# Scores and softmax of the windowed attention issued one half step earlier in the fused kernel

## The chip, the cores and the metric

The kernel runs on one core of a Trainium2 chip. Engines: TensorE (PE; its weight loads are listed as PEld), VectorE (DVE), ScalarE (ACT), GpSimd (POOL), SyncE (SP, which issues most DMAs). The metric is the device time of one execution in microseconds, as the median of several runs.

## The reference

A sliding-window attention, a dense layer with x - tanh(x), and a mixture of 8 experts in which each row goes to one expert:

```python
# q, k, v: (4, 8, 576, 64)
scores = (q @ k.T) / sqrt(64);  mask: 0 <= i - j < 64
attn = softmax(scores, axis=-1)          # row max subtracted, sum + 1e-9
x = (attn @ v) as (2304, 512) rows
h = x @ w_in                             # (512, 2048)
x = (h - tanh(h)) @ w_out                # (2048, 512)
# experts: unit rows of x against unit embeddings, / tau, argmax, softmax gate
out[mask] = gate[mask] * (relu(x[mask] @ w1[e]) @ w2[e])   # w1 512x1024, w2 1024x512
```

## The kernel before

Every product in fp32 accuracy is made of three matmuls of a high and a low part (`products`). The work has two phases: attention with the dense layer (to about 530 us), then the experts.

**Attention** comes in 48 groups. A group is one window of three 64-row blocks of one pair of heads. Its stages are, with their engines: `transpose_qk` (PE, line 1181) turns q and k; `evacuate` (DVE, 861 to 867) copies the turned q into the block-diagonal `qbd`, copies the last key block of the window before to the front of `kT` where the window does not start a sequence (the carry, 865), and copies the three new key blocks (867); `score` (PE, 1192) multiplies them; `mask_max` (DVE, 872) adds the mask and takes the maximum; `exp` (ACT, 654); `pad_sum` and `invert` (DVE, 879, 883); `normalise` (POOL, 521); `transpose_p` (PE, 1203); `copy_pT` (ACT, 661); `attend` (PE, 1219); `copy_x` (ACT, 670); `split_x` (POOL, 530 and 532) makes the high and low part of x.

**The dense layer** is done in 6 blocks of 384 rows. A block has 16 steps, c = 0 to 15, each of 128 hidden columns. In a step TensorE does `first_product(c)` (12 matmuls, x by w_in) and `second_product(c-2)` (9 matmuls, g by w_out). Between them `tanh` (ACT, 703), `less_tanh` (DVE, 954), `high_g` (ACT, 710) and `low_g` (DVE, 958) make g = h - tanh(h) and its two parts. `high_g` waits until the second product that used the same buffer is done.

**The first 8 groups** run before the dense layer. The other 40 are woven into its steps by hand. Each step has two slots: `pieces(s)` after the first product and `pieces(s + 1)` after the second. On VectorE and ScalarE the same slots are after `less_tanh` or `tanh`, and after `low_g` or `high_g`. Group g begins in a slot given by `first_slot`: every third slot for groups 8 to 15, every fourth for 16 to 47, and for the latter it is always the second slot of an even step. In that slot stand its transposes and its evacuation. The later stages stand a fixed number of slots (a lag) behind: score and mask_max at `LAG_SCORE` = 2, exp at 3, pad, reciprocal and normalise at 4, transpose_p at 6, attend and copy_x at 7, split_x at 8. Each engine executes its list in order; semaphores between engines make it wait where something is not there. Within one slot TensorE's order is attend, transpose_p, score, transpose_qk, of different groups. A `score` waits for `qk_evacuated`, which is raised by the key copy (867).

From the second block on VectorE also does the dot products of the router (`dot`, line 975) at the end of steps 3 to 11, four in an odd and one in an even step. In step 14 TensorE ranks rows (`rank`), in step 15 GpSimd scatters slots.

Of the kernel before, what the change touches and what calls it, by code (L numbers as in the profile page):

```python
# [14 lines left out]
BANK = 512  # L15
WINDOW = 64
MASKED = -1.0e30
LAG_SCORE, LAG_TURN, LAG_ATTEND = 2, 6, 7


def wait(eng, semaphore, value):
# [13 lines left out]
def build(nc, q, k, v, w_in, w_out, emb, tau, w1, w2, out):  # L35
# [30 lines left out]
    with ExitStack() as ctx:  # L66
# [254 lines left out]
        def begun(s, lag):  # L321

            return begins.get(s - lag)
# [171 lines left out]
        def _(pool):  # L495
# [23 lines left out]
            def normalise(g):  # L519
                pool.wait_ge(inverted, g + 1)  # L520
                pool.tensor_tensor(sm[g % 4][:], sm[g % 4][:], rr[:, g % 4, :].unsqueeze(2).broadcast_to((P, GB, P)),  # L521
                                   ALU.mult).then_inc(normed, 1)

            def split_x(g):

                n, kk, a = g // FIRST, pair_of(g), g % 2
                high, raw, low = (x[:, kk, n % 2, a, :] for x in (xh, xraw, xl))
                done = g if g < FIRST // 2 else g - FIRST // 2
                pool.wait_ge(x_copied, g + 1)
                pool.tensor_copy(high, raw).then_inc(x_high, 1)  # L530
                pool.wait_ge(x_high, done + 1)
                pool.tensor_tensor(low, raw, high, ALU.subtract).then_inc(x_split, 1)
# [48 lines left out]
                    split_x(j - 6)  # L581

            def pieces(s):
                if (g := begun(s, LAG_SCORE + 2)) is not None:
                    normalise(g)
                if (g := begun(s, LAG_ATTEND + 1)) is not None:
                    split_x(g)

            for n in range(NBLK):
                for c, s in steps(n):  # L590
                    if n == 0 and c + 2 < FC:
                        split_w_in(c + 2)
                    pieces(s)
                    pieces(s + 1)
                    if n == 0 and c in (3, 5):
                        constants(1 if c == 3 else 2)
                    if n == 0 and c == 6:
                        pool.wait_ge(en_squared, 1)
                        pool.tensor_tensor(enroot[:], en1[:, 0:1], power[0:E, 0:1], ALU.pow).then_inc(en_rooted, 1)
                    if n > 0 and c == 8:  # L600
                        pool.wait_ge(squared, ST * n)
                        pool.tensor_tensor(norm[:], ss[:], power[:], ALU.pow).then_inc(rooted, 1)
                    if n > 0 and c == 15:
                        scatter_slots(n - 1)
# [45 lines left out]
        def _(act):  # L650
            def exp(g):
                act.wait_ge(maxed, g + 1)
                for u in range(GB):
                    last = act.activation(sm[g % 4][:, u, :], sm[g % 4][:, u, :], ACT.Exp, bias=nmx[:, g % 4, u:u + 1],
                                          scale=-1.0, accum_out=rs[:, g % 4, u:u + 1])
                last.then_inc(exped, 1)

            def copy_pT(g):
                act.wait_ge(p_transposed, g + 1)
                wait(act, attended, g - 1)  # L660
                act.copy(pT[g % 2][:], psP(g)).then_inc(pT_copied, 1)

            def copy_x(g):
                n, kk, a = g // FIRST, pair_of(g), g % 2
                act.wait_ge(attended, g + 1)

                wait(act, h_ready, FC * (n - 1))
                for h in range(2):
                    rows = slice(h * D, (h + 1) * D)
                    last = act.copy(xraw[rows, kk, n % 2, a, :].rearrange("p (g c) -> p g c", g=GB),  # L670
                                    psO(g)[rows, :, h * WINDOW:(h + 1) * WINDOW])
                last.then_inc(x_copied, 1)
# [15 lines left out]
                    copy_x(j - 5)  # L688

            def pieces(s):  # L690
                if (g := begun(s, LAG_SCORE + 1)) is not None:
                    exp(g)
                if (g := begun(s, LAG_TURN)) is not None:
                    copy_pT(g)
                if (g := begun(s, LAG_ATTEND)) is not None:
                    copy_x(g)
# [35 lines left out]
            for n in range(NBLK):  # L732
                for c, s in steps(n):
                    if n > 0 and c == 2:
                        copy_acc(n - 1)
                    tanh(n, c)
                    pieces(s)
                    high_g(n, c)
                    pieces(s + 1)
                    if n == 0:  # L740
                        high_w_out(c)
                    if n > 0 and c in (3, 5, 7):
                        square(n - 1, (c - 3) // 2)
                    if n > 0 and c == 14:
                        exp_gate(n - 1)
# [97 lines left out]
        def _(dve):  # L843
# [10 lines left out]
            def evacuate(g):  # L854
                i, hp = g % 2, pair_of(g)
                dve.wait_ge(qk_transposed, g + 1)

                wait(dve, scored, g - 1)
                for h in range(2):
                    rows = slice(h * D, (h + 1) * D)  # L860
                    dve.tensor_scalar(qbd[i][rows, :, h, :], psT(g)[rows, :, 0:WINDOW], float(D) ** -0.5, None, ALU.mult)
                wait(dve, scored, g if g % 2 else g - FIRST + 2)
                if window_of(g) % GP:
                    carries[0] += 1
                    dve.tensor_copy(kT[hp][:, 0, :], kT[hp][:, GB, :]).then_inc(carried, 1)
                    dve.wait_ge(carried, carries[0])
                dve.tensor_copy(kT[hp][:, 1:1 + GB, :], psT(g)[:, :, WINDOW:P]).then_inc(qk_evacuated, 1)

            def mask_max(g, units):

                for u in units:
                    last = dve.tensor_tensor_reduce(sm[g % 4][:, u, :], psS(g)[:, u, :], (mask0 if window_of(g) % GP == 0 and u == 0 else mask)[:],
                                                    -1.0, -2.0 * MASKED, ALU.add, ALU.min, nmx[:, g % 4, u:u + 1])
                if units[-1] == GB - 1:
                    last.then_inc(maxed, 1)

            def pad_sum(g):
                dve.wait_ge(exped, g + 1)
                dve.tensor_scalar(rse[:, g % 4, :], rs[:, g % 4, :], 1e-9, None, ALU.add).then_inc(sum_padded, 1)

            def invert(g):
                dve.wait_ge(sum_padded, g + 1)
                dve.reciprocal(rr[:, g % 4, :], rse[:, g % 4, :]).then_inc(inverted, 1)  # L883
# [41 lines left out]
            def pieces(s):  # L925
                if (g := begun(s, 0)) is not None:
                    evacuate(g)
                if (g := begun(s, LAG_SCORE + 2)) is not None:
                    pad_sum(g)
                    invert(g)  # L930
                if (g := begun(s, LAG_SCORE)) is not None:
                    dve.wait_ge(scored, g + 1)
                    dve.wait_ge(p_transposed, g - 3)
                    mask_max(g, [0, 1, 2])
# [84 lines left out]
            for n in range(NBLK):  # L1019
                for c, s in steps(n):  # L1020
                    if n > 0 and c == 2:
                        copy_acc(n - 1)
                    less_tanh(n, c)
                    pieces(s)
                    low_g(n, c)
                    pieces(s + 1)
                    if n > 0 and c == 13:
                        choose(n - 1, dots[:])
                    if n > 0 and c == 15:
                        place(n - 1)  # L1030
                    if n > 0 and 3 <= c <= 11:

                        done = (c - 3) // 2 * 5 + (0 if c % 2 else 4)
                        for r in range(done, done + (4 if c % 2 else 1)):
                            dot(n - 1, r // ST, r % ST)
                    if n == 0:
                        low_w_out(c)
                    if n == 0 and c == 6:
                        scale_emb()
                    if n == 0 and c == 8:  # L1040
                        dve.wait_ge(en_transposed, 1)
                        dve.tensor_copy(enT[:].rearrange("p k e -> p (k e)"), banks[:, 7, 0:KC * E]).then_inc(en_ready, 1)
# [7 lines left out]
            def low_first_w1(pieces):  # L1050
                low_pieces(w1raw, w1h, w1l, ds(0, 1), w1_high, w1_split, 0, pieces)
# [421 lines left out]
```

## Time and profile before

| | us |
|---|---|
| median of 3 runs | 849.17 (849.06 to 849.85) |
| the profiled execution: its time, its span | 849.17, 847.0 |
| TensorE busy | 804.4 (95%) |
| VectorE busy | 468.0 (55%) |
| ScalarE busy | 368.0 (43%) |
| GpSimd busy | 200.5 (24%) |

The page cuts the span in 40 slices. TensorE is at nine tenths or more in nearly all of them, save the first, the change from the dense layer to the experts near 550 us, and the last. Durations of rows that follow each other on TensorE overlap, since matmuls are pipelined: what a matmul takes from the engine is the distance between the starts of two rows. The shares of VectorE and the others say little, for it counts only whether TensorE waits for them.

### The profile page before, as it was taken

The numbers are of one execution on the slowest core, as the hardware profiler recorded it, in microseconds if no ns is written. First come the engines' busy times: TensorE is split into PE (matmuls) and PEld (weight loads), VectorE is DVE, ScalarE is ACT, GpSimd is POOL, SyncE is SP. The second block draws the span as 40 slices with busy tenths as digits, with TensorE's granted clock in tenths as the row PEclk, the third lists the DMA queues.
The fourth block names the chain that finished last, engine by engine and source line by source line (L and its number), as shares of the span: only waits on it lengthen the run. The fifth ranks groups of instructions, "written<-read, shape, count | busy, mean of one in ns | idle before, by whom it ended". The sixth has DMA issues, their size and how long they took to land. (4 is left out here: it accounts for less than half of the span.)

```text
span 847.0 us, 16644 instructions
## 1 busy us (share of the span) xinstructions
PE 804.4 (95%) x4680; PEld 694.5 (82%) x4681; DVE 468.0 (55%) x1399; ACT 368.0 (43%) x910; POOL 200.5 (24%) x276
## 2 busy tenths in 40 slices
PE   7899999999999999999999998399999999999992
PEld 6888888888888888888889997278888888888871
DVE  7666645765577567756763665645443251654322
ACT  4554544433443344344442324246444442664333
POOL 4457621223122312131211001301111111111111
PEclk9999999999999999999999999599999999999995
DMA  9972123322332233223206211056271523466110
GB/s 176 238 232 67 40 51 100 76 61 49 99 79 56 50 100 85 52 50 100 69 14 224 75 38 38 27 202 221 73 236 47 185 93 121 152 236 225 49 47 17
DMA packets 106310, 87.87 MB, mean 104 GB/s; under 512 B 79012, under 2 KB 80169, under 8 KB 106242
## 3 DMA queue, kind: packets, MB, share of 16 engines
q1 hardware_dynamic: 98386, 74.92, 30.6%
q0 software_dynamic: 4624, 11.32, 4.4%
q10 hardware_dynamic: 3232, 0.79, 0.5%
q8 instruction: 35, 0.57, 0.3%
q14 instruction: 33, 0.27, 0.1%
HBM read 152.87 MB, written 11.46 MB: 194 GB/s over the span
## 5 line engine op out<-in xcount | busy, mean ns | idle before, releaser
L1259 PE MATMUL banks<-xh,win_h 128*128 128x384 f32 x384 | 135.6, 353 | 0.9 <-issue 0.9
L1260 PE MATMUL banks<-xl,win_h 128*128 128x384 f32 x384 | 129.1, 336 | 0.0
L1261 PE MATMUL banks<-xh,win_l 128*128 128x384 f32 x384 | 129.1, 336 | 0.0
L958 DVE TENSOR_TENSOR gl<-gf,gh 128x384 fp32r<-128x384 f32 x96 | 55.6, 579 | 132.0 <-ACT gh L710 132.0
L1259 PE MATMUL banks<-wout_h,gh 128*128 128x512 f32 x288 | 117.5, 408 | 0.0
L1260 PE MATMUL banks<-wout_l,gh 128*128 128x512 f32 x288 | 114.0, 396 | 0.0
L1261 PE MATMUL banks<-wout_h,gl 128*128 128x512 f32 x288 | 113.5, 394 | 0.0
L703 ACT ACTIVATE gf<-banks 128x384 f32<-128x384 f32 x96 | 47.2, 492 | 152.4 <-PE banks L1261 151.9
L521 POOL TENSOR_TENSOR sm<-sm,rr 128x384 f32<-128x384 f32 x48 | 47.6, 991 | 270.0 <-DVE rr L883 270.0
L710 ACT CAST gh<-gf 128x384 fp32r<-128x384 f32 x96 | 49.2, 512 | 130.4 <-PE banks L1261 112.9
L1136 DVE TENSOR_TENSOR hTl<-banks,hTh 128x512 fp32r<-128x512 f32 x50 | 32.3, 687 | 92.0 <-ACT hTh L807 91.9
L1259 PEld LDWEIGHTS banks<-xh,win_h 128*128 128x128 f32 x384 | 72.3, 188 | 2.0 <-issue 1.1
L1259 PE MATMUL banks<-w1h,xgh 128*128 x176 | 70.5, 401 | 2.7 <-DVE xgl L1144 2.7
L1260 PEld LDWEIGHTS banks<-xl,win_h 128*128 128x128 f32 x384 | 72.4, 188 | 0.7
L1261 PEld LDWEIGHTS banks<-xh,win_l 128*128 128x128 f32 x384 | 72.1, 188 | 0.0
L1259 PE MATMUL banks<-w2h,hTh 128*128 x176 | 70.4, 400 | 0.9 <-DVE hTl L1136 0.9
L954 DVE TENSOR_TENSOR gf<-banks,gf 128x384 f32<-128x384 f32 x96 | 53.3, 555 | 30.0 <-ACT gf L703 29.9
L1261 PE MATMUL banks<-w1h,xgl 128*128 x176 | 69.0, 392 | 0.0
L1261 PE MATMUL banks<-w2h,hTl 128*128 x176 | 69.0, 392 | 0.0
L1260 PE MATMUL banks<-w1l,xgh 128*128 x176 | 68.8, 391 | 0.0
L1260 PE MATMUL banks<-w2l,hTh 128*128 x176 | 68.8, 391 | 0.0
L1261 PEld LDWEIGHTS banks<-wout_h,gl 128*128 128x128 f32 x288 | 54.1, 188 | 12.3
(192 smaller groups left out, 1504.1 us busy)
## 6 DMA issues: line engine op xcount, KB each, us to landing
w1raw<-in_moe_w_dram SPq DMA_DIRECT2D x104, 512.0 KB
w2raw<-in_moe_w_dram SPq DMA_DIRECT2D x104, 512.0 KB
x2T<-unit_embeddings SPq DMA_DIRECT2D x20, 256.0 KB, 3.6
junk<-unit_embeddings SPq DMA_DIRECT2D x20, 256.0 KB, 3.6
x_rows<-x SPq DMA_DIRECT2D x6, 768.0 KB, 5.2
wout_raw<-in_moe_w_out_dram SPq DMA_DIRECT2D x4, 1024.0 KB, 6.8
win_raw<-in_moe_w_in_dram SPq DMA_DIRECT2D x3, 1024.0 KB, 9.8
vw<-in_v_dram SPq DMA_DIRECT2D x16, 192.0 KB, 3.2
```

The costliest lines, as they stand in the source:

```text
L521: pool.tensor_tensor(sm[g % 4][:], sm[g % 4][:], rr[:, g % 4, :].unsqueeze(2).broadcast_to((P, GB, P)), ALU.mult).then_inc(normed, 1)
L703: act.activation(gf[c % 2][:], psH[c % 2], ACT.Tanh).then_inc(tanh_ready, 1)
L710: act.copy(gh[c % 2][:], gf[c % 2][:]).then_inc(g_high, 1)
L954: dve.tensor_tensor(gf[c % 2][:], psH[c % 2], gf[c % 2][:], ALU.subtract).then_inc(g_ready, 1)
L958: dve.tensor_tensor(gl[c % 2][:], gf[c % 2][:], gh[c % 2][:], ALU.subtract).then_inc(g_split, 1)
L1136: dve.tensor_tensor(hTl[:, part, :], psHT[half].rearrange("p (k t) -> p k t", k=KC), hTh[:, part, :], ALU.subtract).then_inc(hT_split, 1)
L1259: pe.matmul(to, sh, mh, start=start, stop=False)
L1260: pe.matmul(to, sh, ml, start=False, stop=False)
L1261: return pe.matmul(to, sl, mh, start=False, stop=stop)
```

## The change

`LAG_SCORE` goes from 2 to 1. The lags that were written as sums with it become the numbers 3, 2 and 3; they were 4, 3 and 4. So the score with mask_max, the exp, and pad, reciprocal and normalise of groups 8 to 47 all stand one slot sooner in the lists of their engines. transpose_p, attend and what follows keep their slots. The number of instructions is the same on each engine.

```diff
-LAG_SCORE, LAG_TURN, LAG_ATTEND = 2, 6, 7
+LAG_SCORE, LAG_TURN, LAG_ATTEND = 1, 6, 7
...
-                if (g := begun(s, LAG_SCORE + 2)) is not None:
+                if (g := begun(s, 3)) is not None:
                     normalise(g)
...
-                if (g := begun(s, LAG_SCORE + 1)) is not None:
+                if (g := begun(s, 2)) is not None:
                     exp(g)
...
-                if (g := begun(s, LAG_SCORE + 2)) is not None:
+                if (g := begun(s, 3)) is not None:
                     pad_sum(g)
                     invert(g)
```

TensorE, kernel before, end of an odd step in block 1. The rows with `wout` are a second product, L1203 are the probability transposes of the group before, L1192 the score, and the rows with `win` the next first product:

```order
442 L1260 MATMUL banks<-wout_l,gh 128x512
443 L1261 MATMUL banks<-wout_h,gl 128x512
444 L1203 MATMUL banks<-ident,sm 128x128 x3
445 L1192 MATMUL banks<-kT,qbd 128x128 x3
446 L1259 MATMUL banks<-xh,win_h 128x384
447 L1260 MATMUL banks<-xl,win_h 128x384
```

The changed kernel, the middle of the same step, where the first product ends and the second begins:

```order
433 L1260 MATMUL banks<-xl,win_h 128x384
434 L1261 MATMUL banks<-xh,win_l 128x384
435 L1192 MATMUL banks<-kT,qbd 128x128 x3
436 L1259 MATMUL banks<-wout_h,gh 128x512
437 L1260 MATMUL banks<-wout_l,gh 128x512
```

The score has gone ahead of the nine matmuls of the second product, so that one first product alone lies between a group's transposes and its score; the probability transposes stay behind the second product.

VectorE, kernel before, an even step of block 2. L954 is `less_tanh`, L958 `low_g`, L861 to L867 the evacuation, L879 and L883 pad and reciprocal of the group before, L975 a router dot:

```order
520 L954 TENSOR_TENSOR gf<-banks,gf 128x384
521 L958 TENSOR_TENSOR gl<-gf,gh 128x384
522 L861 TENSOR_SCALAR qbd<-banks 64x3x64 x2
523 L865 COPY kT<-kT 128x64
524 L867 COPY kT<-banks 128x192
525 L879 TENSOR_SCALAR rse<-rs 128x3
526 L883 RECIPROCAL rr<-rse 128x3
```

The same step of the changed kernel:

```order
513 L954 TENSOR_TENSOR gf<-banks,gf 128x384
514 L879 TENSOR_SCALAR rse<-rs 128x3
515 L883 RECIPROCAL rr<-rse 128x3
516 L958 TENSOR_TENSOR gl<-gf,gh 128x384
517 L861 TENSOR_SCALAR qbd<-banks 64x3x64 x2
518 L865 COPY kT<-kT 128x64
519 L867 COPY kT<-banks 128x192
```

Pad and reciprocal, for which GpSimd's normalisation waits, have gone from behind the evacuation to before `low_g`. In the odd step the three mask-and-max instructions go from behind `low_g` to before it in the same way, so that the dots follow `low_g` at once.

## Rows read from the trace of the kernel before

**Rows 1.** Busy time by stretches, first and last of four; last columns: granted clock, DMA.

```profile
115.00:198.00 83.00, 83.00 (x530) 73.23 (x529) 53.04 (x186) 35.92 (x114) 16.60 (x25) 1.00 0.32 78
366.00:450.00 84.00, 84.00 (x529) 74.13 (x528) 51.96 (x188) 34.85 (x108) 20.16 (x30) 1.00 0.27 73
```

**Rows 2.** The list of waits, TensorE: us in total, times, longest.

```profile
PE banks L1192 <- DVE kT L867: 2.5, 4, 1.1
```

**Rows 3.** Order of time around group 27: start, duration, engine, line.

```profile
217.51 0.49 PE L1181 MATMUL banks<-ident,qk 128*128 128x128 f32 x3
...
217.76 0.51 ACT L710 CAST gh<-gf 128x384 fp32r<-128x384 f32 x1 [0.68 <-PE banks L1261]
...
218.31 0.56 DVE L958 TENSOR_TENSOR gl<-gf,gh 128x384 fp32r<-128x384 f32 x1 [2.31 <-ACT gh L710]
...
219.51 0.20 DVE L865 COPY kT<-kT 128x64 f32<-128x64 f32 x1
...
219.74 0.36 DVE L867 COPY kT<-banks 128x192 f32<-128x192 f32 x1
219.78 0.33 PE L1261 MATMUL banks<-xh,win_l 128*128 128x384 f32 x1
...
219.95 0.39 PE L1259 MATMUL banks<-wout_h,gh 128*128 128x512 f32 x1
```

**Rows 4.** Order of time: a score that waited, then one that did not.

```profile
40.81 0.36 DVE L867 COPY kT<-banks 128x192 f32<-128x192 f32 x1
...
41.23 0.94 PE L1192 MATMUL banks<-kT,qbd 128*128 128x128 f32 x6 [1.13 <-DVE kT L867]
41.92 0.42 PE L1259 MATMUL banks<-xh,win_h 128*128 128x384 f32 x1
...
56.95 0.83 PE L1192 MATMUL banks<-kT,qbd 128*128 128x128 f32 x6
57.54 0.42 PE L1259 MATMUL banks<-xh,win_h 128*128 128x384 f32 x1
```

**Rows 5.** Line 865, the carry copy: duration in ns min/median/max.

```profile
L865 DVE COPY kT<-kT x32: 195/195/1242, 8.3 to 428.5; 128x64 f32<-128x64 f32 x32
```

**Rows 6.** Order of time around group 26, which has no carry.

```profile
207.10 0.49 PE L1181 MATMUL banks<-ident,qk 128*128 128x128 f32 x3
...
209.14 0.36 DVE L867 COPY kT<-banks 128x192 f32<-128x192 f32 x1
...
209.54 0.39 PE L1259 MATMUL banks<-wout_h,gh 128*128 128x512 f32 x1
```

**Rows 7.** Order of time, GpSimd and VectorE side by side.

```profile
85.74 1.29 POOL L541 TENSOR_TENSOR win_l<-win_raw,win_h 128x512 fp32r<-128x512 f32 x1
...
85.87 1.57 DVE L958 TENSOR_TENSOR gl<-gf,gh 128x384 fp32r<-128x384 f32 x1 [1.64 <-ACT gh L710]
```

**Rows 8.** Order of time: block 0 to 57.68, then a step with router dots.

```profile
55.57 0.55 DVE L954 TENSOR_TENSOR gf<-banks,gf 128x384 f32<-128x384 f32 x1
...
56.49 0.83 POOL L521 TENSOR_TENSOR sm<-sm,rr 128x384 f32<-128x384 f32 x1 [1.87 <-DVE rr L883]
...
57.26 0.34 POOL L530 CAST xh<-xraw 128x192 fp32r<-128x192 f32 x1
...
57.68 0.61 POOL L532 TENSOR_TENSOR xl<-xraw,xh 128x192 fp32r<-128x192 f32 x1
...
233.72 0.28 DVE L872 CUSTOM_DVE_ANT_0 sm<-banks,mask 128x128 f32<-128x128 f32 x1
...
234.35 0.70 DVE L975 CUSTOM_DVE_ANT_0 banks<-x,junk 128x512 f32<-128x512 f32 x1
...
237.70 0.55 DVE L954 TENSOR_TENSOR gf<-banks,gf 128x384 f32<-128x384 f32 x1
...
238.32 0.49 PE L1181 MATMUL banks<-ident,qk 128*128 128x128 f32 x3
...
239.12 0.56 DVE L958 TENSOR_TENSOR gl<-gf,gh 128x384 fp32r<-128x384 f32 x1 [0.87 <-ACT gh L710]
```

## The prediction

> **What bounds the kernel now.** I read the busy time by stretches first. From 115 to 450 us TensorE is busy in 83.00 of 83.00 and 84.00 of 84.00 us, at a granted clock of 1.00, in each of the four stretches [rows 1]. All but the first few of the 40 moved groups lie there. In such a stretch a microsecond taken from VectorE, ScalarE or GpSimd brings nothing, and a microsecond for which TensorE waits is added to the whole. Then the list of waits: TensorE has waited for the key copy (line 867) only 4 times, 2.5 us in all, all at the start of the program [rows 2]. The change cannot remove a wait that is not there. The question is only whether it makes new ones, so the third view is the order of time around one group.
>
> **Where a score stands now and where it will stand.** For group 27 the three q/k transposes start at 217.51. ScalarE's rounding of g (line 710) waits for the second product just before them and starts at 217.76; VectorE's subtraction (958) follows at 218.31; only then come the evacuations, the last being the carry copy (865) at 219.51 and the key copy (867) at 219.74 for 0.36, so the keys are there at 220.10, T+2.59 if T is the start of the transposes. TensorE meanwhile does one first product and starts the next second product at 219.95, T+2.44 [rows 3]. Before, the score came a whole second product later, and that was its slack. With a lag of 1 it stands exactly at T+2.44. The whole chain from 217.76 on hangs on TensorE's own second product, so it moves along with TensorE and does not catch up.
>
> **Part 1, the late groups with a carry.** Need 2.44, have 2.59: 0.15 us short. What does a wait really cost? The score of group 8 is a wait of the same kind: the copy at 40.81 for 0.36 ends at 41.17, the score starts at 41.23, so 0.06 from release to start. It then took 0.69 until the next product (41.92), against 0.59 for a score that did not wait (56.95 to 57.54): another 0.10, for its weight load is no longer hidden behind an earlier matmul [rows 4]. So 0.15 + 0.06 + 0.10 = 0.31 per group. Which groups? Carries are made in all windows that do not start a sequence, 32 of 48 groups [rows 5]. Of the 32 groups 16 to 47, 24 have one. Four of those are spared: 25 and 41, because the rank matmuls of step 14 stand between; 16, because an attention product does; and 17, whose second product ends half a microsecond sooner. That leaves 20: 20 x 0.31 = **6.2 us**. Lower end 20 x 0.15 = 3.0 (no release time, no exposed load), upper end 20 x 0.40 = 8.0.
>
> **Part 2, the late groups without a carry.** For group 26 the transposes start at 207.10, the key copy ends at 209.14 + 0.36 = 209.50, TensorE comes at 209.54 [rows 6]. With 0.06 for the release that is 0.02 late at most. There are 7 such (33 is behind rank matmuls). Between 0 and the 0.10 of the exposed load plus 0.02; I take 0.05: **0.35 us**, ends 0 and 0.8.
>
> **Part 3, the eight early groups.** Their rhythm is three slots, not four, and an attention product often stands ahead of the score, which gives VectorE time. Group 8 waits where it waited before (in step 1 there is no second product between the two places). By the same comparison about three of the other seven are short by up to 0.3. GpSimd, though, moves there too: it now stops for the reciprocal before a split of w_in instead of after, so its long subtractions fall elsewhere. I take **0.8 us**, ends 0 and 8 x 0.31 = 2.5.
>
> **Part 4, the matmuls' neighbours.** Score and probability transposes stood together; now each stands alone. A product that follows such a block has 0.42 for its first matmul [rows 4] against 0.33 within a product [rows 3], so a change-over costs some 0.09, but the pair already had one inside it. I take 0.01 per group, **0.3 us**, ends 0 and 32 x 0.09 = 2.9.
>
> **Part 5, what goes off VectorE, ScalarE and GpSimd's way.** The mask-and-max now comes before the low part of g in the odd step. It waits for the score, ends long before the rounding of g is done, since that waits for TensorE's second product, and costs nothing. The exp goes from before the rounding of g to after it, and now stands ahead of the copy of the transposed probabilities: that copy is later by the three exps, but is needed only a whole first product after its transposes, which takes most of the 2.44 us above; no wait. Pad, reciprocal and normalisation come half a step sooner, where they were never late. SyncE's loads wait for transposes and attention products, whose places stay. All at nothing, hidden behind TensorE; what is late next is the key copy itself.
>
> **The sum.** 6.2 + 0.35 + 0.8 + 0.3 = 7.65 us. Against the profiled execution's own 849.17 us (span 847.0), which is also the median of the runs, that is 856.8 us. Nothing after 450 us can win it back: the last block and the expert phase hang on the end of this one.
>
> **A rule that speaks against the change.** At 85.74 GpSimd started a subtraction of 1.29 us and at 85.87 VectorE's low part of g, usually 0.56, took 1.57: it stood until GpSimd was through [rows 7]. Now place the new GpSimd work of a step with router dots. Without the masks (233.72 to 234.35, 0.63) ahead of them, the dots end 0.63 sooner, so the less-tanh subtraction, at 237.70 for the transposes at 238.32, starts at T-1.25. From such a subtraction, with pad and reciprocal right behind it, normalisation starts 0.92 later (55.57 to 56.49), the rounding of x 0.77 after that (57.26) and the subtraction of x 0.42 later still (57.68): T-0.33, T+0.44 and T+0.86. The low part of g starts at T+0.80 [rows 8]. It is ahead of GpSimd's subtraction by 0.06 us, and behind the rounding (0.34 long) by 0.02. In the trace of before GpSimd does all of this after the key copy.
> The Trainium skill, SBUF — State Buffer, section "SBUF: two separate sides", says that VectorE (with two SBUF inputs, or in a mode that uses both ports) and GpSimd take one pair of ports as an exclusive lock: who starts first keeps it for the whole instruction and the other waits. By that, the order at T+0.80 decides between nothing and a full block; the trace agrees in the 1.57 us row.
>
> **The rivals.**
> - *GpSimd gets there first.* If its subtraction of x (0.61 in rows 8) starts before the low part of g, that and all behind it is late by about 0.55. There are 20 groups behind a step with four dots (steps 4 to 12 of blocks 1 to 4): 20 x 0.55 = 11 us more, 867.8 us. Decided by 0.06 us, but the distances in question repeat to 0.02 in the trace. Chance 0.09 for all of them, 0.08 for a part (about 860 to 864).
> - *The release comes sooner than the record ends, and the load stays hidden.* Then 0.08 of the 0.15 is gone and neither 0.06 nor 0.10 is paid: 20 x 0.07 = 1.4, nothing in part 2 and 3: about 850.6 us, not slower in a measurement. It decides at a release 0.1 before the end of the copy's record. For it: ends of records hold a tail. Against: the two starts in rows 4. Chance 0.08.
> - *The groups do not come short at all, or shorter GpSimd waits in block 0 give something back*: the exp out of the way of the rounding of g, say. But TensorE has no idle time to give back [rows 1, 2], so a gain above 0.2% needs something that I don't see in the profile: 0.02, about 847.
>
> **How the numbers follow.** Forecast 0.73, 856.8 us, its own range 853.0 to 860.5 from the ends above. With the partial block included the range reaches 864.0, at the lower side 852.0; left out are 0.09 + 0.08 + 0.02. A measurement of this kernel can tell about 0.2% (1.7 us) from no change. Slower: 0.73 + 0.09 + 0.08 = 0.90; same 0.08; faster 0.02.
>
> **What would show it.** In the profile of the changed kernel the list of waits should have TensorE at line 1192 waiting for the key copy (867) over 20 times, each about 0.2 us or below, some 4 to 5 us in all (the exposed load does not count as a wait there). TensorE's busy time in blocks 1 to 4 should fall just under the full stretch; two steps should take 10.7 us with a carry and 10.4 without. The median of line 958 should stay 0.56; if it is near 1, GpSimd's lock is in it. If line 1192 shows no wait, parts 1 and 2 are wrong. If a carry copy (865) is often over 0.20, GpSimd has hit that instead.

## The result, and the profile after

| | us |
|---|---|
| the kernel before, median | 849.12 (848.97 to 849.85) |
| the changed kernel, median of 4 runs | 864.46 (864.05 to 864.90) |
| ratio | 1.0181 (95%: 1.0169 to 1.0193) |
| the profiled execution of the changed kernel: its time, its span | 865.77, 863.6 |

The kernel became 15.3 us slower. The sign was forecast, and the cause of one half of it. The size was twice the 7.65 us of the sum, and it lies 0.5 us above the range. What the sum lacked is the subject of the rest.

The list of TensorE's waits in the changed kernel, us in total, times and longest. The second row answers to [rows 2], where it was 2.5 us in 4 times; the third was not there before.

```profile
PE banks L1343 <- DMA tabs<-slots,rows: 10.6, 1, 10.6
PE banks L1192 <- DVE kT L867: 10.3, 22, 1.1
...
PE banks L1259 <- ACT x L719: 1.3, 4, 0.3
```

The score (1192) waits for the key copy (867) over 20 times, as forecast, but twice as much in all; and a second product (1259) waits four times for ScalarE's copy of the accumulator (719).

The busy time by stretches, for [rows 1]:

```profile
115.00:200.00 85.00, 83.21 (x519) 71.55 (x519) 54.70 (x186) 35.87 (x114) 15.45 (x24) 1.00 0.28 72
...
370.00:460.00 90.00, 87.85 (x554) 75.81 (x552) 56.27 (x199) 36.74 (x116) 19.19 (x28) 1.00 0.22 55
```

TensorE, full before, now lacks about 2% of each stretch. The granted clock is 1.00 in these stretches, as before, so no part of the loss there is clock.

To see where the loss falls I measured from the start of one group's transposes (line 1181) to the next group's. Those of groups 16 and 47 start here (order of time, TensorE alone):

```profile
103.46 0.49 PE L1181 MATMUL banks<-ident,qk 128*128 128x128 f32 x3
...
441.70 0.49 PE L1181 MATMUL banks<-ident,qk 128*128 128x128 f32 x3
```

That is 338.24 us; before it was 324.48 (102.00 to 426.48), so 13.76 us lie there. From group 8 to 16, in block 0, it is 66.85 us against 64.48; but group 8 started 0.9 sooner in this execution, so that group 16 is late by 1.5.

Now group 29, in a step with router dots (order of time, each engine listed by itself; T = 244.50):

```profile
243.90 0.55 DVE L954 TENSOR_TENSOR gf<-banks,gf 128x384 f32<-128x384 f32 x1
...
244.50 0.49 PE L1181 MATMUL banks<-ident,qk 128*128 128x128 f32 x3
...
244.82 0.83 POOL L521 TENSOR_TENSOR sm<-sm,rr 128x384 f32<-128x384 f32 x1 [8.58 <-DVE rr L883]
...
245.30 0.77 DVE L958 TENSOR_TENSOR gl<-gf,gh 128x384 fp32r<-128x384 f32 x1 [0.55 <-ACT gh L710]
245.59 0.67 POOL L530 CAST xh<-xraw 128x192 fp32r<-128x192 f32 x1
245.99 0.71 DVE L861 TENSOR_SCALAR qbd<-banks 64x192 f32<-64x192 f32 x2
246.71 0.28 DVE L865 COPY kT<-kT 128x64 f32<-128x64 f32 x1
247.03 0.36 DVE L867 COPY kT<-banks 128x192 f32<-128x192 f32 x1
247.44 0.94 PE L1192 MATMUL banks<-kT,qbd 128*128 128x128 f32 x6 [0.34 <-DVE kT L867]
248.13 0.48 PE L1259 MATMUL banks<-wout_h,gh 128*128 128x512 f32 x1
```

GpSimd's normalisation (521) runs from T+0.32 to T+1.15. The low part of g (958) starts at T+0.80 as forecast, but takes 0.77 instead of 0.56; the rounding of x (530) behind it takes 0.67 instead of 0.34. The carry copy (865) too is 0.28 instead of 0.20. So the keys are there at T+2.89, not T+2.59, and the score starts at T+2.94. The next product comes 0.69 after it, so the 0.10 of the exposed weight load is real.

Taking each distance between two transposes and subtracting its length before (10.41 us; 10.83 where rank matmuls stand, 11.00 after group 16) gives this ledger of the changed kernel:

| groups 16 to 47 | count | excess each, us | in all |
|---|---|---|---|
| carry, no dots ahead (19, 27, 43) | 3 | 0.31 to 0.33 | 1.0 |
| carry, after dots (one of them, 31: 0.93) | 13 | 0.60 | 8.2 |
| no carry, after dots | 5 | 0.29 | 1.4 |
| first step of blocks 1 to 4 (18, 26, 34, 42) | 4 | 0.66, 0.48, 0.99, 1.00 | 3.1 |
| no carry, no dots (35) | 1 | 0.07 | 0.1 |
| the others (16, 17, 25, 33, 41) | 5 | 0 | 0 |

These are the 31 distances of the 13.76 us. Group 47, the last, has none behind it; its rows stand as those of group 46 (score at T+2.95), so that it adds another 0.6. "After dots" are the groups whose transposes stand in a step behind one with four router dots.

### The profile page after: what moved, and what is told of

Same layout as the page of the kernel before. It is cut to its first block and busy times, and to the rows that moved or that the text cites. A ratio compares the mean times of both kernels' runs of the same rounds, so it can differ in the third digit from the quotient of the medians.

```text
span 863.6 us, 16644 instructions
## 1 busy us (share of the span) xinstructions
PE 811.5 (94%) x4680; PEld 694.1 (80%) x4681; DVE 473.6 (55%) x1399; ACT 367.6 (43%) x910; POOL 199.9 (23%) x276
## 5 line engine op out<-in xcount | busy, mean ns | idle before, releaser
L958 DVE TENSOR_TENSOR gl<-gf,gh 128x384 fp32r<-128x384 f32 x96 | 59.2, 617 | 130.1 <-ACT gh L710 130.1
L1259 PE MATMUL banks<-wout_h,gh 128*128 128x512 f32 x288 | 119.8, 416 | 1.3 <-ACT x L719 1.3
L521 POOL TENSOR_TENSOR sm<-sm,rr 128x384 f32<-128x384 f32 x48 | 41.7, 869 | 273.3 <-DVE rr L883 273.2
L954 DVE TENSOR_TENSOR gf<-banks,gf 128x384 f32<-128x384 f32 x96 | 53.2, 554 | 34.3 <-ACT gf L703 34.1
L1259 PEld LDWEIGHTS banks<-wout_h,gh 128*128 128x128 f32 x288 | 54.2, 188 | 12.5 <-issue 1.7
```

The costliest lines, as they stand in the source:

```text
L954: dve.tensor_tensor(gf[c % 2][:], psH[c % 2], gf[c % 2][:], ALU.subtract).then_inc(g_ready, 1)
L958: dve.tensor_tensor(gl[c % 2][:], gf[c % 2][:], gh[c % 2][:], ALU.subtract).then_inc(g_split, 1)
L1259: pe.matmul(to, sh, mh, start=start, stop=False)
```

## The experiments

Each kernel was timed beside the kernel before on the same chip. The second number is its ratio to that kernel, with the 95% interval; "over before" in us is the difference of the two medians, which can differ from the ratio by half a microsecond. E1 to E4, E5 to E8 and E9 to E11 ran together.

### E1: pad, reciprocal and normalisation back at lag 4

From the changed kernel, on GpSimd and on VectorE alike:

```diff
-                if (g := begun(s, 3)) is not None:
+                if (g := begun(s, 4)) is not None:
```

> The changed kernel, but pad, reciprocal and normalisation stay at their old lag of 4 slots; score at 1 and exp at 2 as changed. Theory A (GpSimd's normalisation, now next to the low part of g, holds it up by 0.2 us and so the score by 0.3 us in some 19 groups, and the carry copy behind the scatters in two more): line 958 goes back to 0.56 everywhere in blocks 1 to 4, the excess per group from 0.60 to 0.31, and the time falls by about 6 us to 858.4 us. Theory B (the exp's or the matmuls' new places cost it): no change, 864.5 us.

Measured 857.15 us, 1.0095 (1.0078 to 1.0112). The excess of a group with a carry after dots fell from 0.60 to 0.30, without carry from 0.29 to 0.08; groups 16 to 47 took 332.37 us instead of 338.24. In its profile the list of waits has

```profile
PE banks L1192 <- DVE kT L867: 3.0, 5, 1.1
```

5 waits, though some 27 scores come late. A wait on TensorE is counted there from the modelled end of the matmul before, 0.33 after its start, but the next matmul could have started 0.17 after it. A delay of 0.15 hides in that overlap and costs all the same. Theory A holds: GpSimd's place was worth 5.9 us.

### E5: the same, by moving GpSimd alone

```diff
                 pool.wait_ge(inverted, g + 1)
+                if 2 * FIRST <= g < NG - 1:
+                    pool.wait_ge(qk_evacuated, g + 2)
```

> The changed kernel with every place as changed, but for groups 16 on GpSimd's normalisation also waits until the key copy of the next group is done, so that no GpSimd work lies beside the low part of g. Theory A (the pair of ports that GpSimd and VectorE share): line 958 at 0.56, excess per group with a carry 0.31, time some 6 us under the changed kernel, 8.5 to 9.5 us over the one before (857 to 858.5 us). Theory B (pad and reciprocal on VectorE ahead of the low part of g are what delays it): 864.5 us as the changed kernel.

Measured 858.05 us, 1.0110 (1.0093 to 1.0127). Groups 16 to 47 took 332.39 us, as in E1 to 0.02 us, with pad and reciprocal where the change has them. So it is GpSimd's work, not VectorE's two small instructions, that holds up the low part of g.

### E3: pad, reciprocal and normalisation alone, score and exp at their old places

From the changed kernel; the second piece is the exp on ScalarE:

```diff
-LAG_SCORE, LAG_TURN, LAG_ATTEND = 1, 6, 7
+LAG_SCORE, LAG_TURN, LAG_ATTEND = 2, 6, 7
...
-                if (g := begun(s, 2)) is not None:
+                if (g := begun(s, 3)) is not None:
```

> The score at its old lag of 2 and the exp at its old 3; only pad, reciprocal and normalisation come one slot forward, to 3. Theory A: GpSimd still hits the low part of g (line 958 at 0.77 in steps with router dots), but a whole second product lies between the key copy and the score, so TensorE never waits: 849.1 us, same as before. Theory B (GpSimd's place costs time by itself): about 6 us more, 855 us.

Measured 849.42 us, 1.0006 (0.9996 to 1.0015): the same as before. The collision is there, here at group 27 (order of time, VectorE and TensorE; T = 217.55):

```profile
217.55 0.49 PE L1181 MATMUL banks<-ident,qk 128*128 128x128 f32 x3
...
218.35 0.95 DVE L958 TENSOR_TENSOR gl<-gf,gh 128x384 fp32r<-128x384 f32 x1 [1.34 <-ACT gh L710]
...
222.40 0.83 PE L1192 MATMUL banks<-kT,qbd 128*128 128x128 f32 x6
```

The low part of g takes 0.95 (0.72 to 0.74 in the groups after dots, but for 31), the keys come at T+2.99, and it costs nothing, since the score comes at T+4.85. Groups 16 to 47 took 324.48 us, to the hundredth what they took before. A held-up chain costs only where the slack behind it is gone: the change did both at once.

### E2: score and mask-and-max alone

From E1, the exp on ScalarE:

```diff
-                if (g := begun(s, 2)) is not None:
+                if (g := begun(s, 3)) is not None:
```

> Score and mask-and-max alone at the new lag of 1; exp at its old 3, pad, reciprocal and normalisation at their old 4. Theory A: what is left is the key copy that comes too late, 20 groups x 0.31 plus a little, so about 856 us; two further waits go against the kernel before it, those of the second product on the copy of the accumulator (4 x 0.35 us) and of VectorE on ScalarE's rounding of w_out in block 0 (some 2 us), since both stand behind an exp that came forward. Theory B (the score's place alone costs all 15 us): 864 us.

Measured 856.35 us, 1.0085 (1.0068 to 1.0102), 7.7 us over before. Every group with a carry pays 0.30 or 0.31 (31: 0.39), every one without 0.07 to 0.09 but for 26 (0.14). Against E1, groups 16 to 47 lost another 1.40 us, and the waits on the accumulator's copy are gone from the list. This kernel is what parts 1 to 4 of the prediction priced. From group 16 to 47 it took 330.97 us, 6.5 over before, and from 8 to 16, in block 0, 65.01 against 64.48.

### E4: only groups 8 to 15 moved

`begun_either` stands for `begun` where score, mask-and-max, exp, pad and normalisation are issued:

```diff
+        def begun_either(s, lag):
+            early = begun(s, lag)
+            if early is not None and early < 2 * FIRST:
+                return early
+            late = begun(s, lag + 1)
+            return late if late is not None and late >= 2 * FIRST else None
```

> Only the groups 8 to 15, which run in block 0, are moved as in the change; groups 16 to 47 keep the old lags. Theory A: block 0 costs 2.4 us, from scores 9 and 13 that wait over 1 us each for a key copy behind a low part of w_out: 851.5 us. Rival: those waits are made up for in the slack of block 0, and all of the 15 us is in the later groups: 849.1 us.

Measured 850.11 us, 1.0016 (1.0006 to 1.0026), 1.5 us over before, less than expected. Groups 9 and 13 wait for their keys (the added lines push the others 8 down: 1200 is the score, 875 the key copy):

```profile
46.68 0.94 PE L1200 MATMUL banks<-kT,qbd 128*128 128x128 f32 x6 [0.31 <-DVE kT L875]
...
80.86 0.94 PE L1200 MATMUL banks<-kT,qbd 128*128 128x128 f32 x6 [0.94 <-DVE kT L875]
```

### E6 and E9: what the exp pushed back on ScalarE

In the changed kernel the exp now stands ahead of two things: the rounding of w_out (676, block 0), which VectorE needs before it can go on to the next evacuation, and the copy of the accumulator (719), which a second product needs. E6 moves both out from behind it, E9 the first alone.

E9 has only the lines on `high_w_out` of this:

```diff
-                    if n > 0 and c == 2:
-                        copy_acc(n - 1)
                     tanh(n, c)
                     pieces(s)
                     high_g(n, c)
+                    if n > 0 and c == 1:
+                        copy_acc(n - 1)
+                    if n == 0:
+                        high_w_out(c)
                     pieces(s + 1)
-                    if n == 0:
-                        high_w_out(c)
```

> The changed kernel with two ScalarE pieces taken out from behind the exp: the copy of the accumulator stands right after the rounding of g in step 1, and the rounding of w_out in block 0 before the exp. Theory A: the four waits of the second product on the copied accumulator go (4 x 0.35 = 1.4 us), and 0.5 to 1.5 us of block 0: 1.9 to 2.9 us less than the changed kernel, about 862 us. Rival: these waits only hide others, no change, 864.5 us.

E6 measured 864.40 us, 1.0181 (1.0164 to 1.0198): no change, a miss. Block 0 gave back 2.3 us, more than the 0.5 to 1.5 expected (64.56 from group 8 to 16), but groups 16 to 47 took 340.26 us, 2.0 more. In its profile:

```profile
132.42 0.47 ACT L661 COPY pT<-banks 128x384 f32<-128x384 f32 x1
...
132.94 0.57 PE L1219 MATMUL banks<-pT,vw 128*64 128x64 f32 x12 [0.71 <-ACT pT L661]
```

The copy of the transposed probabilities (661), behind the exp and now also behind the accumulator's copy too, ends at 132.89, and the attention product (1219) stands 0.71 us for it; it did not wait there in the changed kernel. The wait was moved, and made longer.

> The changed kernel with one piece of e6 alone: in block 0 ScalarE rounds w_out before the exp, and the copy of the accumulator stays where the change has it. Theory A (in e6 the 2.3 us won in block 0 were lost again because the copy of the accumulator then stood ahead of the copy of the transposed probabilities): 2.3 us less than the changed kernel, 862.1 us. Rival (block 0 differs by chance, with the arrival of w_in): 864.4 us.

E9 measured 864.54 us, 1.0168 (1.0153 to 1.0184), where 862.1 was expected: a miss in the whole time. From group 8 to 16 it took 64.95 us, 1.9 less than the changed kernel, and 338.50 from 16 to 47, as the changed kernel. By the clock of the trace group 16 starts at 103.01 against 103.46, only 0.45 sooner, since group 8 started 1.4 later. The intervals of E9 and the change overlap, so that block 0's part of the total is not settled better than 0.5 to 2 us.

### E7 and E8: the carry copy taken out of the chain

```diff
             def pieces(s):
+                if (g := begun(s, -1)) is not None and g >= 2 * FIRST:
+                    carry(g)
                 if (g := begun(s, 0)) is not None:
                     evacuate(g)
```

`carry(g)` holds the wait, the copy (865) and its semaphore, which `evacuate` then does without.

> As e1 (score 1, exp 2, pad, reciprocal and normalisation at 4), and for groups 16 on the carry copy is made one slot before the transposes, so it no longer stands between them and the key copy. Theory A: the key copy is there at T+2.36 instead of T+2.59, and the 19 to 20 groups with a carry pay 0.07 instead of 0.30: 4.5 us less than e1, about 852.6 us. Rival (what costs is the score's wait as such, not the length of VectorE's chain): 857 us as e1.

> As e2 (score and mask-and-max alone at lag 1), with the carry copy taken out of the chain as in e7. Theory A: nothing is left but some 0.07 us in 27 groups and block 0: 2 to 3 us over the kernel before, about 851.5 us; it cannot be faster than before, since TensorE had no wait in blocks 1 to 4 to win. Rival: the earlier score gains something once it no longer waits: under 848 us.

E7 measured 854.71 us, 1.0072 (1.0055 to 1.0089), 2.4 less than E1, where 4.5 was expected; E8 852.95 us, 1.0048 (1.0031 to 1.0065), 3.4 less than E2, where 4.9 was expected. From group 16 to 47 both took 2.5 less. The direction is right and the size little more than half: a group with a carry went from 0.30 to 0.13, not 0.07, and one without a carry from 0.08 to 0.14. Group 29 of E8 (order of time; T = 240.10; here 871 is the carry copy, 864 the key copy, 965 the low part of g, 1188 the transposes and 1199 the score):

```profile
239.97 0.19 DVE L871 COPY kT<-kT 128x64 f32<-128x64 f32 x1
240.10 0.49 PE L1188 MATMUL banks<-ident,qk 128*128 128x128 f32 x3
...
240.97 0.56 DVE L965 TENSOR_TENSOR gl<-gf,gh 128x384 fp32r<-128x384 f32 x1 [0.81 <-ACT gh L710]
...
242.17 0.36 DVE L864 COPY kT<-banks 128x192 f32<-128x192 f32 x1
...
242.58 0.94 PE L1199 MATMUL banks<-kT,qbd 128*128 128x128 f32 x6
```

The carry copy starts before T, but the low part of g starts at T+0.87 where it started at T+0.80, in all groups from 18 on but 22; there it starts at T+1.23 in both kernels, and 0.5 is lost. Why it is later was not tried. Without the carry the keys come at T+2.43 and the score still waits. Neither beats the kernel before: in blocks 1 to 4 that one had nothing to win.

### E10: does it add up?

The changed kernel with the exp set back to 3, by the same edit as in E2: score at 1, exp at 3, pad, reciprocal and normalisation at 3.

> Score at 1, exp at its old 3, pad, reciprocal and normalisation at the changed 3: what e2 lacks of the change but for the exp. Theory A, by adding up the pieces: 856.3 (e2) + 5.6 (low part of g behind the normalisation in 19 groups) + 0.7 (carry copy behind it after the scatters in two groups), so 862.6 us, without the 1.4 us of the accumulator's copy. Rival: the exp, which now ends later beside pad and reciprocal in the same slot, holds them up and so moves GpSimd off the low part of g: 857 to 858 us.

Measured 865.14 us, 1.0176 (1.0161 to 1.0192): 15.2 us over before, where 14.0 was expected; the rival had the opposite sign. Groups after dots behave as in the change (0.61). But those with a carry and without dots ahead, 0.31 to 0.33 in the change, now have 0.69 to 0.71. Group 27 (T = 222.60):

```profile
221.67 0.17 DVE L879 TENSOR_SCALAR rse<-rs 128x3 f32<-128x3 f32 x1 [0.59 <-ACT sm L654]
...
222.13 0.83 POOL L521 TENSOR_TENSOR sm<-sm,rr 128x384 f32<-128x384 f32 x1 [6.48 <-DVE rr L883]
...
223.33 0.60 POOL L532 TENSOR_TENSOR xl<-xraw,xh 128x192 fp32r<-128x192 f32 x1
223.40 0.95 DVE L958 TENSOR_TENSOR gl<-gf,gh 128x384 fp32r<-128x384 f32 x1 [1.34 <-ACT gh L710]
```

Pad and reciprocal wait for the exp in the same slot, so GpSimd's work is later, and its last piece, the subtraction of x (532), starts 0.07 before the low part of g, which then takes 0.95. This is the rival of the prediction, GpSimd's subtraction getting there first by a few hundredths, though in the steps without dots, and with its price: 0.39 instead of the 0.55 put down. That price stood in the trace of the kernel before, beside a row that the prediction used, the subtraction at 57.68:

```profile
57.75 0.95 DVE L958 TENSOR_TENSOR gl<-gf,gh 128x384 fp32r<-128x384 f32 x1 [1.34 <-ACT gh L710]
```

### E11: block 0 begun one slot sooner, in the kernel before

```diff
-            return 3 * i + 1 if n == 0 else SLOTS * n + 4 * i - 7
+            return 3 * i if n == 0 else SLOTS * n + 4 * i - 7
```

> The kernel before with the groups 8 to 15 begun one slot sooner (slots 0, 3, 6, ... instead of 1, 4, 7, ...), so that the score of group 8, which waits 1.13 us in step 1 for want of a second product ahead of it, has less to wait. Theory A: up to 1.0 us less than before, 0.1%. Rival: with the other parity the scores of block 0 meet the splits of w_in on GpSimd elsewhere, and it is as before or up to 1 us slower.

Measured 850.63 us, 1.0009 (1.0000 to 1.0018), 0.7 over before: the rival. The wait of group 8 got shorter, but two transposes now wait for a maximum (2.0 us). Nothing won.

## Why the prediction was half right

**What bounds the kernel, and parts 1 and 2: right.** E2 is the experiment for them. 0.31 per group with a carry was forecast, 0.30 or 0.31 measured; 0.05 without, 0.07 to 0.09 measured; the groups spared were those named. Release and exposed load were rightly taken from the one score that had waited [rows 4]. That the whole sum, 7.65 us, meets E2's 7.7 to a tenth is in part luck: E2's interval is 1.4 us wide to either side, part 2 cost about 0.6 instead of 0.35, and part 4, a change-over between matmuls, cannot be seen where it stands alone (of the five groups that do not come late none has a longer distance).

**Part 3, block 0: too small, and for a reason only half seen.** 0.8 was put down; the early groups alone cost 1.5 us (E4), at groups 9 and 13. Two of the moved things meet there. The exp, now ahead of the rounding of w_out on ScalarE, lets VectorE's low part of w_out (950) start only after GpSimd's split of w_in (541), and then it takes 1.59. In E1, where normalisation keeps its old place ahead of that split, 950 starts first and takes 0.78. The changed kernel, then E1 (order of time):

```profile
77.69 1.29 POOL L541 TENSOR_TENSOR win_l<-win_raw,win_h 128x512 fp32r<-128x512 f32 x1
...
77.94 1.59 DVE L950 TENSOR_TENSOR wout_l<-wout_raw,wout_h 128x512 fp32r<-128x512 f32 x1 [1.33 <-ACT wout_h L676]
```

```profile
77.71 0.78 DVE L950 TENSOR_TENSOR wout_l<-wout_raw,wout_h 128x512 fp32r<-128x512 f32 x1 [1.20 <-ACT wout_h L676]
...
78.03 1.62 POOL L541 TENSOR_TENSOR win_l<-win_raw,win_h 128x512 fp32r<-128x512 f32 x1
```

The distances behind groups 9 and 13 are 1.35 and 1.21 us over before in the change, 0.53 and 0.31 in E1, 0.45 and 0.21 in E9. So taking back either piece alone removes most of it there, though E9's whole time does not show the gain.

**Part 5, "all at nothing": wrong for one thing.** It asked what the exp does to the copy behind it in the same slot, but not to the piece of the step that follows: the accumulator's copy. That cost 4 x 0.35 = 1.4 us (E2 against E1).

**The paragraph on GpSimd: the right danger, and the step that failed.** It said that the new GpSimd work would clear the low part of g by hundredths. The reckoning was made backwards from the transposes, T, and took the 0.63 of the masks out of VectorE's list. But the score had left the same stretch of TensorE's list: between the odd step's second product and T there were probability transposes, score and first product, and now there is no score. Group 29's probability transposes (1203) and its first dot (975), before (T = 238.32) and changed (T = 244.50):

```profile
232.44 0.49 PE L1203 MATMUL banks<-ident,sm 128*128 128x128 f32 x3
...
234.35 0.70 DVE L975 CUSTOM_DVE_ANT_0 banks<-x,junk 128x512 f32<-128x512 f32 x1
```

```profile
239.28 0.49 PE L1203 MATMUL banks<-ident,sm 128*128 128x128 f32 x3
...
240.56 0.69 DVE L975 CUSTOM_DVE_ANT_0 banks<-x,junk 128x512 f32<-128x512 f32 x1
```

The probability transposes, right behind that second product, started at T-5.88 and now start at T-5.22: T comes 0.66 sooner after them. The first dot was at T-3.97 and is at T-3.94: the gain of the masks is eaten up. So the less-tanh subtraction starts at T-0.60 (243.90), not T-1.25, and the normalisation at T+0.32, not T-0.33. The work that meets the low part of g is not the last piece of GpSimd's three, but the first, in 19 groups (not 20: the last one counted would be a group 48): 14 x 0.30 + 5 x 0.21 = 5.3 us. With the accumulator's copy (1.4), the carry copies of groups 34 and 42 (0.7; below) and 0.2 for group 31 this is 7.6 us, which brings E2's 7.7 to 15.3. That sum closes no better than about 1 us, for block 0 is in it only as far as E2 has it (65.01 us from group 8 to 16, the change 66.85, but there group 8 started 1.6 sooner). Group 31 is one where the distances did not repeat to 0.02: its less-tanh subtraction was at T-0.27 already before, normalisation now starts at T+0.67, and the low part of g takes 1.04.

**What fell outside.** Groups 34 and 42 were not singled out. There GpSimd is late from the scatters of step 15, starts the normalisation at 301.04, and the carry copy behind it takes 0.55:

```profile
301.04 0.84 POOL L521 TENSOR_TENSOR sm<-sm,rr 128x384 f32<-128x384 f32 x1
...
301.40 0.55 DVE L865 COPY kT<-kT 128x64 f32<-128x64 f32 x1
...
302.40 0.94 PE L1192 MATMUL banks<-kT,qbd 128*128 128x128 f32 x6 [0.40 <-DVE kT L867]
```

**The rivals.** "GpSimd gets there first, for a part" had 0.08 with 860 to 864 us; the result is that case, by another piece of GpSimd and a little above its range. The release that comes sooner and the gain did not happen. Of the signs named for it one misled: the median of line 958 did stay at 0.56, which would have been read as "no lock", for 72 of its 96 instructions take 0.60 or less. The other, a carry copy over 0.20, did show (0.28). The rows by group show it plainly; the list of waits is as coarse as the median (E1). The range was not the plain sum of the ends either: 3.0 to 14.2 us would have been 852.2 to 863.4, not 853.0 to 860.5.

## What to carry to other kernels

An instruction that is moved earlier takes its time out of one stretch and puts it into another: when the places of other engines' work are reckoned from a landmark, add up what left the stretch on every engine's list, the landmark's own above all. Before a chain loses its slack, look at what else is moved next to it: GpSimd beside VectorE was free as long as a product lay behind (E3) and cost 5.9 us once it did not. On a queue that runs full, the list of waits and the medians by line are too coarse; the distance between two like instructions, group by group, finds every tenth of a microsecond.

## What was not expected of the hardware

A GpSimd instruction and a VectorE subtraction with two inputs hold each other up both ways: 0.83 of normalisation made a 0.56 subtraction 0.77, and that subtraction made a 0.34 rounding 0.67. The hold is shorter than the overlap of the rows: rows overlap by 0.35 and the loss is 0.21. The difference is 0.13 to 0.16 in all thirteen traces, wherever VectorE's low part of g started while a normalisation, a rounding or a subtraction of GpSimd ran and that one alone held it up. So the loss can be reckoned from two rows: overlap less some 0.15. Not every GpSimd row does it. The power of three elements per partition (602) let such a subtraction pass at its usual 0.56, four times in the kernel before:

```profile
170.18 0.90 POOL L602 TENSOR_TENSOR norm<-ss,power 128x3 f32<-128x3 f32 x1
...
170.38 0.56 DVE L958 TENSOR_TENSOR gl<-gf,gh 128x384 fp32r<-128x384 f32 x1 [1.33 <-ACT gh L710]
```

A score that waited took 0.66 to 0.70 until the next product, one that had not 0.58 or 0.59, in all the kernels that were read by group, so that a delay of a few hundredths costs 0.07 to 0.14. The Trainium skill, SBUF — State Buffer, section "SBUF: two separate sides", has the later one stand until the earlier one is through; the trace bears out the exclusion and its direction (E10, E5), but the end of a GpSimd row comes some 0.14 after VectorE is let in, and beside the power of 128x3 no hold shows at all, where the page speaks of the whole instruction.
